# One core, attention, routed experts and a feed-forward layer: register reads, root steps, output copies and closing waits are reordered

## The reference, cut to what matters

```python
# attention: B, H, S, D = 4, 8, 768, 48
for t in range(S):
    state = alpha[:, :, t, :, None] * state + einsum('bhd,bhe->bhde', k[:, :, t], v[:, :, t])
    y[:, :, t] = einsum('bhd,bhde->bhe', q[:, :, t], state)
x = y transposed to (3072 tokens, 384)
# top-1 experts: E, F = 8, 1024
xn, en = x / (norm(x) + 1e-6), expert_emb / (norm(expert_emb) + 1e-6)
logits = xn @ en.T / tau; expert_idx = argmax(logits); gate_w = softmax(logits)[expert_idx]
out[mask_e] = gate_w * (relu(x[mask_e] @ w1[e]) @ w2[e])
# feed-forward: d_ff = 2048
h = out @ w_in; g = where(h > 0, h, exp(min(h, 0)) - 1); result = g @ w_out
```

## Time and profile before

| | us |
|---|---|
| median of 3 runs | 910.74 |
| all runs | 911.87, 910.74, 910.71 |
| the profiled execution | 911.53 |
| its span, first to last instruction | 909.9 |
| PE busy in it | 879.2 |

### The profile page before, as it was taken

One profiled execution on the slowest core, in us unless ns is written; L12 is line 12 of the kernel. 1 busy time (PEld: TensorE's weight loads), 2 busy tenths in 40 slices (PEclk: granted clock), 3 DMA queues, 4 the chain that ended last, 5 costly groups with the idle time before them and its releaser, 6 DMA issues. The chain is left out here.

```text
span 909.9 us, 16294 instructions
## 1 busy us (share of the span) xinstructions
PE 879.2 (97%) x5725; PEld 777.8 (85%) x5725; DVE 436.1 (48%) x828; ACT 320.5 (35%) x709; POOL 267.9 (29%) x279
## 2 busy tenths in 40 slices
PE   8999999889999999999999999999999999999995
PEld 5787888678989989999888899999999899899894
DVE  7887888872222222322325545445445445445442
ACT  4565646623222222232332223223223223223221
POOL 3114244447545754564807201001001001001001
PEclk9999999999999999999999999999999999999998
DMA  9965774688878789746807102002002002000000
GB/s 155 163 120 116 155 151 96 212 280 268 259 243 280 246 259 302 238 137 189 220 20 235 42 1 70 1 1 70 1 1 70 1 0 70 1 1 35 1 1 35
DMA packets 140975, 107.92 MB, mean 119 GB/s; under 512 B 103354, under 2 KB 129074, under 8 KB 140898
## 3 DMA queue, kind: packets, MB, share of 16 engines
q0 software_dynamic: 25696, 66.09, 22.8%
q1 hardware_dynamic: 115202, 40.79, 20.2%
HBM read 89.51 MB, written 17.35 MB: 117 GB/s over the span
## 5 line engine op out<-in xcount | busy, mean ns | idle before, releaser
L1406 POOL DMA_INDIRECT out<-of,idi x24 | 23.6, 983 | 370.1 <-DVE of L1492 305.4
L1226 PE MATMUL bank<-WX,hdTh 128*128 (+1 forms) x496 | 129.5, 342 | 3.0 <-DVE hdTl L1279 1.7
L1450 PE MATMUL bank<-xT_h,wi_h 128*128 128x512 f32 x288 | 114.3, 397 | 0.0
L1450 PE MATMUL bank<-xT_l,wi_h 128*128 128x512 f32 x288 | 113.7, 395 | 0.0
L1450 PE MATMUL bank<-xT_h,wi_l 128*128 128x512 f32 x288 | 113.5, 394 | 0.0
L1532 DVE TENSOR_SCALAR em<-ee 128x512 f32<-128x512 f32 x96 | 44.7, 465 | 136.0 <-ACT ee L1510 133.8
L1510 ACT ACTIVATE ee<-bank 128x512 f32<-128x512 f32 x96 | 57.3, 597 | 147.2 <-PE bank L1450 144.2
L1212 PE MATMUL bank<-WX,xdTh 128*128 (+1 forms) x372 | 99.7, 403 | 3.3 <-ACT xdTh L1252 1.5
L1513 ACT ACTIVATE g_h<-gg 128x512 fp32r<-128x512 f32 x96 | 60.6, 632 | 116.3 <-DVE gg L1537 114.6
L1150 POOL TENSOR_TENSOR WX<-raw_w,WX 128x3072 fp32r<-128x3072 f32 x14 | 95.5, 6821 | 17.8 <-DMA WX<-moe_w 12.9
L1541 DVE TENSOR_TENSOR g_l<-gg,g_h 128x512 fp32r<-128x512 f32 x96 | 69.9, 728 | 60.2 <-ACT g_h L1513 59.3
(11 more groups left out here) (215 smaller groups left out, 1387.2 us busy)
## 6 DMA issues: line engine op xcount, KB each, us to landing
WX<-moe_w POOLq DMA_DIRECT2D x14, 1536.0 KB, 9.9
raw_w<-moe_w POOLq DMA_DIRECT2D x14, 1536.0 KB, 8.6
xd<-sorted_x SPq DMA_DIRECT2D x31, 193.0 KB, 5.3
sorted_y<-yd SPq DMA_DIRECT2D x31, 192.5 KB, 4.6
xg<-sorted_y SPq DMA_DIRECT2D x6, 770.0 KB, 4.4
nat_a<-alpha SPq DMA_DIRECT2D x32, 144.0 KB, 3.3
nat_k<-k SPq DMA_DIRECT2D x32, 144.0 KB, 3.5
nat_q<-q SPq DMA_DIRECT2D x32, 144.0 KB, 3.6
```

The lines of the kernel that those rows point to most:

```text
L1226: last = pe.matmul(y_out(t)[:, 0:DM], hdT[a][:, k * P:(k + 1) * P], WX[:, bass.ds(off + (b * WE + KD * F + k * DM), DM)], start=(k == 0 an ...
L1450: last = pe.matmul(bank[4 + i % 2][:, :], a[:, k, w], b[:, k, :], start=(k == 0 and m == 0), stop=(k == KD - 1 and m == 2))
```

## The change

- PE reads a tile's position once, by a step `K` that stands ahead of the waits of `HT0` of the tile before; `M10`, `M11` and `M2` take it from there. Before, each of the three read it on its own.
- On POOL, `U0` moves from ahead of `PM` and the root steps to behind them, still ahead of the scatters of the last batch.
- On DVE, the last six steps of the ladder (those of `dst`) move behind `Ye` of tile 0 and `He0`, `He1` of tile 1.
- Output tiles 0 and 2 are copied by ACT and 1 and 3 by DVE; before, the other way round.
- The waits for the last output scatters move from the end of POOL's program to the end of SP's.
- In the last group `O14` leaves its tile 3 out, and this part is computed between tiles 1 and 2 of `O15`.

```diff
                 if b == PARTIAL and r == 0:
-                    out_ += [("U0", 1), ("PM", b)] + roots + [("SC", b * C + j) for j in range(C)]
+                    out_ += [("PM", b)] + roots + [("U0", 1)] + [("SC", b * C + j) for j in range(C)]
...
-        acE = Steps(sem("acE"), ["E0", "G0"] + [f"O{t}" for t in range(1, GT, 2)]
+        acE = Steps(sem("acE"), ["E0", "G0"] + [f"O{t}" for t in range(0, GT, 2)]
...
-        veE = Steps(sem("veE"), ["M0", "G0"] + [f"O{t}" for t in range(0, GT, 2)] + ["L0"]
+        veE = Steps(sem("veE"), ["M0", "G0"] + [f"O{t}" for t in range(1, GT, 2)] + ["L0"]
...
+            places = {}
             def position(t):
-                return pe.value_load(kth[0:1, t:t + 1], min_val=0, max_val=E - 1) if t >= EARLY else 0
+                if t not in places:
+                    k = pe.value_load(kth[0:1, t:t + 1], min_val=0, max_val=E - 1) if t >= EARLY else 0
+                    places[t] = (k, pe.snap(k % 2 * (2 * WE)) if t >= EARLY else 0)
+                    places.pop(t - 2, None)
+                return places[t]
...
-            for t in range(GT):
-                po.wait_ge(s_out[t], 16 * GROUPS)
...
+                if i == K2 - 2 and n == GROUPS - 1:
+                    return [of_tile(i, t) for t in range(GT - 1)][-1]
                 if i == K2 - 1 and n == GROUPS - 1:
-                    acE.wait(pe, f"G{i}", n)
                     for t in range(GT):
-                        for m, (a, b) in enumerate(three):
-                            if m == 2 and t == 0:
-                                veE.wait(pe, f"L{i}", n)
-                            last = pe.matmul(bank[t][:, 0:DM], a[i % 2][:, t * P:(t + 1) * P], b[:, i, :], start=False, stop=(m == 2))
+                        if t == GT - 2:
+                            of_tile(K2 - 2, GT - 1)
+                        last = of_tile(i, t)
...
             for g in range(1, GROUPS):
                 sp_tokens(sp, g)
+            for t in range(GT):
+                sp.wait_ge(s_out[t], 16 * GROUPS)
...
-            climb(ve, "vector", n_emb, len(ladder))
-            d(("Ye", 0), ("He0", 1), ("He1", 1), ("Ye", 1), ("Xe", 2), ("Xe", 3))
+            climb(ve, "vector", n_emb, n_tiles)
+            d(("Ye", 0), ("He0", 1), ("He1", 1))
+            climb(ve, "vector", n_tiles, len(ladder))
+            d(("Ye", 1), ("Xe", 2), ("Xe", 3))
...
-            d(("M10", 2), ("XT", 3), ("M11", 2))
+            d(("K", 2), ("M10", 2), ("XT", 3), ("M11", 2))
             for t in range(EARLY, TILES):
-                d(("HT0", t), ("HT1", t))
+                d(("K", t + 1), ("HT0", t), ("HT1", t))
```

More of the change, by code:

```diff
@@ L1180, in pe_d @@
         def pe_d(pe):
+            places = {}
             def position(t):
-                return pe.value_load(kth[0:1, t:t + 1], min_val=0, max_val=E - 1) if t >= EARLY else 0
-            def half_of(k):
-                return pe.snap(k % 2 * (2 * WE)) if not isinstance(k, int) else k % 2 * (2 * WE)
+                if t not in places:
[3 more added lines that the diff above has]
+                return places[t]
             def step(name, t):
@@ L1198, in step @@
                     i = int(name[2])
-                    k_ = position(t)
+                    k_, off = position(t)
                     upper_only, rest = name[3:] == "u", name == "M10" and t == 0
@@ L1204, in step @@
                         acD.wait(pe, f"Re{i}", t - 1)
-                    off = half_of(k_)
                     for m, (a, b) in enumerate(((0, 0), (0, 1), (1, 0))):
@@ L1239, in do @@
                 for name, t in steps:
-                    if t < TILES:
+                    if t < TILES and name == "K":
+                        position(t)
+                    elif t < TILES:
                         ins = step(name, t)
@@ L1403, in po_e @@
                 for t in range(GT):
-                    (acE if t % 2 else veE).wait(po, f"O{t}", g + 1)
+                    (veE if t % 2 else acE).wait(po, f"O{t}", g + 1)
                     po.wait_ge(s_id, g + 1)
@@ L1454, in emit, with of_tile @@
                 three = ((g_h, wo_h), (g_h, wo_l), (g_l, wo_h))
+                def of_tile(c, t):
+                    for m, (a, b) in enumerate(three):
+                        if m == 0:
+                            acE.wait(pe, f"G{c}", n)
+                        if m == 2:
+                            veE.wait(pe, f"L{c}", n)
+                        ins = pe.matmul(bank[t][:, 0:DM], a[c % 2][:, t * P:(t + 1) * P], b[:, c, :], start=False,
+                                        stop=(c == K2 - 1 and m == 2))
+                    return ins
+                if i == K2 - 2 and n == GROUPS - 1:
+                    return [of_tile(i, t) for t in range(GT - 1)][-1]
                 if i == K2 - 1 and n == GROUPS - 1:
-                    acE.wait(pe, f"G{i}", n)
                     for t in range(GT):
-                        for m, (a, b) in enumerate(three):
-                            if m == 2 and t == 0:
-                                veE.wait(pe, f"L{i}", n)
-                            last = pe.matmul(bank[t][:, 0:DM], a[i % 2][:, t * P:(t + 1) * P], b[:, i, :], start=False, stop=(m == 2))
+                        if t == GT - 2:
+                            of_tile(K2 - 2, GT - 1)
+                        last = of_tile(i, t)
                         if t < GT - 1:
@@ L1475, in emit @@
                         if i == 0 and m == 0:
-                            (acE if t % 2 else veE).wait(pe, f"O{t}", n)
+                            (veE if t % 2 else acE).wait(pe, f"O{t}", n)
                         last = pe.matmul(bank[t][:, 0:DM], a[i % 2][:, t * P:(t + 1) * P], b[:, i, :],
```

## The result

| | before | changed |
|---|---|---|
| median | 910.73 us (6 runs, 910.31 to 911.87) | 914.64 us (6 runs, 913.71 to 915.07) |
| profiled execution | 911.53 | 914.13 |
| its span | 909.9 | 912.5 |

The ratio is 1.0040, with a 95% interval of 1.0028 to 1.0052: slower by 3.9 us (2.6 to 4.7). The forecast was 914.6.

The account below looks back on a forecast made before the run. PE was taken as the bound, busy 879.2 of 909.9 us. The terms summed to +3.9 us, added to the median of 910.74 for 914.6 us; the 8-in-10 range was 906.2 to 917.

Parts of the forecast that it names:

- U0's loads: Stage A into D: loads issued 5.1 us later hold up the last scatter and tile 2's gather; +4.7 us.
- What would show it: List of signs expected in the profile after, such as load issue near 185.6 and XT of tile 2 not before 208.
- Rival (1): Stage A into D: scatters aren't held up, zero blocks gate, no hole or lower clock; -4.2, 906.5 us; chance 0.25.
- Ladder: DVE's last six steps, stage A into D: M2 of tile 1 starts 1.7 us earlier, but the gather gates; 0.
- Clock: Behind PE's 6.3 us hole before XT of tile 2: PE falls to the lower clock; +2.5 us.
- rival (2): At PE's hole before XT of tile 2: hole under 4.3 us or later fall, clock holds; 912.1 us; chance 0.13.
- Positions: PE's waits on issue at M10 of tile 3 and M2 of the last tile but one shrink; together -1.1 us.
- Copies: First group of E: the wait on DVE's step moves ahead of tile 3, one matmul goes before it; -0.2 us.
- Tail: Last output group: O15's first tile and POOL's four scatters come earlier, with ACT's faster copy; -0.6 us.
- Closing waits: Program end: POOL reaches its DRAIN about 0.45 us after its last DMA in place of 1.9; -1.4 us.

Follow-up runs that it names:

- e2: The kernel before with only U0 moved behind PM and the root steps; ratio 1.0103, +9.5 us against before on its chip.
- g1: The kernel before with only the positions read once, ahead of the waits; ratio 0.9967, -3.0 us against before on its chip.
- U0 first: The changed kernel with U0 put back ahead of PM and the roots; ratio 0.9949, -4.7 us against before; run again, 0.9947, -4.9 us.

## Why the prediction was right

- **U0's loads.** The mechanism held at every link: loads at 185.75 (forecast 185.6), DMA engines full from 187 to 204 (187 to 204), the gate at 205.1 (205.3), XT of tile 2 at 208.12 (208.6). The term was +4.7 and measured +4.2. "What would show it" named each of these rows. One reason was too narrow: it let the scatters wait behind the loads in POOL's own queue, but the zero blocks of SP's queue waited as long and landed last, at 205.1. Rival (1) had them land as early as before. The full engines account for both.
- **Ladder.** M2 of tile 1 at 197.74 (197.9), its end at 202.14 (202.3), and nothing of it in the time: right. Most of the 1.9 us comes from the roots (1.2 at M10 of tile 1), 0.7 from the ladder.
- **Clock.** The price, +2.5, measured 2.5 (9.34 against 6.82 from XT to HT of tile 2). The condition was wrong: "4.3 us later", and with it "one of 4 would not be". The clock fell 2.2 us after PE stopped, and in other kernels after waits of 3.5, 2.6 and 0.9 us. One fall at the end of the program gave the delay of that one fall, not a limit. So rival (2), "the clock holds", got more chance than its reason was worth. That PE falls to 1.2 GHz after idling and must work before it is at 2.4 GHz again, as the Trainium skill has it (TensorE: Matmul & The Clock Gate, "The HAM clock gate"), agrees with these rows: 0.50 from 2.2 us after PE stopped until 6.5 us after it went on.
- **Positions** -1.1, measured -1.4. The idle times went from 0.36 to 0 and from 1.25 to 0.50 as forecast, but the ends of matmuls in a profile are modelled: from start to start, M10 of tile 3 follows HT of tile 2 by 1.02 us before (210.70 to 211.72) and by 0.41 after (217.46 to 217.87), so 0.6 were won there. **Copies** -0.2: from the end of H1 to the second product's second part 2.33 before (492.51 to 494.84), 2.14 after (497.76 to 499.90). **Tail** -0.6: from PE's last end to POOL's last DMA 3.16 before, 2.54 after. These two as forecast.
- **Closing waits** -1.4, measured -1.9 in the traces and -1.8 (-1.0 to -2.6) alone: mis-sized. I took the DRAIN's 4.8 us from its own start; they count from POOL's last DMA instruction, and its start costs nothing.

The sum of the measured terms is 4.2 + 2.5 - 1.4 - 0.2 - 0.6 - 1.9 = +2.6, just the difference of the two profiled executions. My sum was +3.9, and against the profiled execution it was 1.3 too high: 0.5 in the loads, 0.3 in the positions, 0.5 in the closing waits, all in one direction. Added to the median it met the median to 0.04 us. That is chance: the profiled execution of before lay 0.8 above its median, that of after 0.5 below. Why the medians differ by 1.3 more than the profiles is not shown. The sign and the mechanism don't hang on it, the hit to 0.04 does. That executions of one code can differ at this gate is likely: closing waits alone, with the code of before there, had a wait and a fall that the profile of before had not.

## What to carry to other kernels

A step that issues DMAs carries its bytes with it: before moving it behind something short on its engine, ask how full the DMA engines are between its old and its new place, and what with a deadline arrives behind it; here 4.5 us of idle DMA engines were given up for 1 us of an engine that wasn't last. A wait removed just ahead of a gate that others set is no gain, and the hole that it makes can have a price of its own through the clock.

## What the runs showed of the hardware

- POOL's DRAIN ends 4.8 us after its last scatter instruction in all eleven kernels where it is queued at once, and 4.8 us after its own start in the three (before, e2, g1) where a wait for the landing stands ahead of it.
- A wait of PE of 0.9 us, with one of 0.8 us right behind it, was followed by 3.4 us at the lower clock. A wait of 1.7 us in the kernel before was not. PE's steps in stage A are the same in all kernels: no fall in the profile of the kernel before, four in that of U0 first on its chip.
- A gather that took 2.4 us to land took 7.1 behind 3 MB of loads from another queue, and a zero block 11.2 in place of 4.9. In these runs the queues shared the engines, and a small DMA wasn't served first.
